# Linear attention whose state is summed in one PSUM bank, its chunks worked through two at a time

## What is computed

```python
# attention: batch 2, heads 8, seq 768, head_dim 64
state = gamma * state + k[t] (outer) v[t]          # one 64x64 state per batch and head
y[t]  = 1/sqrt(64) * q[t] @ state                  # gamma = 1 - 2**(-5-head)
x = y laid out as 1536 tokens x 512
# first feed-forward part, d_ff 2048
h = x @ w_in;  x = (h * sigmoid(1.702 h)) @ w_out
# second, d_ff 1536
xn = x / rms(x) * rms_g
x  = (silu(xn @ w_gate) * (xn @ w_val)) @ w_out
```

## Time and profile before

| | |
|---|---|
| three runs | 586.87, 587.14, 587.15 us; median 587.14 |
| profiled execution | 587.46 us, of which the span of the core's instructions is 585.6 |
| attention, until the first feed-forward matmul | 0 to 55.26 us |
| feed-forward parts | 55.26 to 585.60 us |
| mean granted clock of TensorE | 0.997 |

### The profile page before, as it was taken

How to read it: one execution, slowest core, us unless ns; L and a number is a source line. 1 busy time by engine, 2 the same in 40 slices (tenths; PEclk the granted TensorE clock), 3 DMA queues, 4 the chain that set the end, 5 groups by cost and what they waited for, 6 DMA issues and landing times.

```text
span 585.6 us, 9221 instructions
## 1 busy us (share of the span) xinstructions
PE 575.1 (98%) x3558; PEld 552.0 (94%) x3558; DVE 356.0 (61%) x472; ACT 307.8 (53%) x533; POOL 169.2 (29%) x187
## 2 busy tenths in 40 slices
PE   6999999999999999999999999999999999999997
PEld 6888999999999999999999999998889999998886
DVE  3599555667334666876426768668764666667332
ACT  1556666744325766654337655563544555564321
POOL 2674444000122452000123453410060544420000
PEclk8999999999999999999999999999999999999999
DMA  8990122321211222322202222223213322223202
GB/s 324 347 315 29 58 69 72 109 86 59 73 37 36 73 73 72 109 73 72 67 8 72 73 73 73 72 73 108 73 37 103 114 72 73 73 72 109 72 0 107
DMA packets 24363, 52.83 MB, mean 90 GB/s; under 512 B 1920, under 2 KB 2048, under 8 KB 24320
## 3 DMA queue, kind: packets, MB, share of 16 engines
q1 hardware_dynamic: 23744, 50.93, 26.9%
q10 hardware_dynamic: 576, 1.32, 0.6%
HBM read 49.09 MB, written 3.15 MB: 89 GB/s over the span
## 4 chain that ended last, share of the span: by engine, by line
PE 95%; DVE 2%; DMA 2%; issue 1%; SPq 0%; ACT 0%
PE bank L470 39%; PE bank L420 17%; PE bank L422 17%; PE bank L423 17%; DMA arena<-attn_in 2%; PE bank L394 1%; PE bank L363 1%; PE bank L388 1%; DVE arena L823 1%; PE bank L373 1%; DVE arena L841 1%; PE bank L511 0%; DVE x_lo L723 0%; DVE w_lo L714 0%; DVE t L736 0%
## 5 line engine op out<-in xcount | busy, mean ns | idle before, releaser
L420 PE MATMUL bank<-x_hi,w_hi 128*128 128x384 f32 x560 | 187.3, 334 | 0.0
L423 PE MATMUL bank<-x_hi,w_lo 128*128 128x384 f32 x560 | 187.1, 334 | 0.0
L422 PE MATMUL bank<-x_lo,w_hi 128*128 128x384 f32 x560 | 187.1, 334 | 0.0
L714 DVE TENSOR_TENSOR w_lo<-raw,w_hi 128x512 fp32r<-128x512 f32 (+2 forms) x148 | 145.9, 1001 | 50.9 <-ACT w_hi L543 50.7
L975 POOL TENSOR_TENSOR raw<-raw 128x256 f32<-128x256 f32 x40 | 31.9, 796 | 324.1 <-DMA raw<-w 324.1
L543 ACT ACTIVATE w_hi<-raw 128x512 fp32r<-128x512 f32 (+2 forms) x148 | 109.0, 763 | 18.5 <-PE bank L423 10.2
L420 PEld LDWEIGHTS bank<-x_hi,w_hi 128*128 128x128 f32 x560 | 105.1, 188 | 0.1
L422 PEld LDWEIGHTS bank<-x_lo,w_hi 128*128 128x128 f32 x560 | 105.1, 188 | 0.1
L423 PEld LDWEIGHTS bank<-x_hi,w_lo 128*128 128x128 f32 x560 | 105.1, 188 | 0.0
L573 ACT ACTIVATE g_hi<-arena 128x768 fp32r<-128x768 f32 x56 | 47.5, 848 | 103.1 <-PE bank L470 103.1
L749 DVE TENSOR_TENSOR g_lo<-arena,g_hi 128x768 fp32r<-128x768 f32 x56 | 55.2, 986 | 75.2 <-ACT g_hi L573 75.2
(11 more groups left out here) (70 smaller groups left out, 591.0 us busy)
## 6 DMA issues: line engine op xcount, KB each, us to landing
raw<-w SPq DMA_DIRECT2D x68, 512.0 KB, 3.5
arena<-attn_in SPq DMA_DIRECT2D x22, 512.0 KB, 6.7
out<-x SPq DMA_DIRECT2D x1, 1536.0 KB, 7.8
out<-x SPq DMA_DIRECT2D x6, 256.0 KB, 2.0
arena<-attn_in ACTq DMA_DIRECT2D x2, 512.0 KB, 8.1
arena<-tables SPq DMA_DIRECT2D x1, 512.0 KB, 6.7
arena<-tables ACTq DMA_DIRECT2D x1, 256.0 KB, 10.6
ident<-ident_in SPq DMA_DIRECT2D x1, 64.0 KB, 11.4
```

The costliest lines, as they stand in the source:

```text
L420: pe.matmul(dst, w_hi[q][:, w], x_hi[:, x], start=start and kk == 0, stop=False, skip_group_check=True)
L422: pe.matmul(dst, w_hi[q][:, w], x_lo[:, x], start=False, stop=False, skip_group_check=True)
L423: mm = pe.matmul(dst, w_lo[q][:, w], x_hi[:, x], start=False, stop=kk == 1, skip_group_check=True)
L714: dve.tensor_tensor(w_lo[q % 3][:, dst], src, w_hi[q % 3][:, dst].bitcast(F32), ALU.subtract)\
```

## The change

- The state is no longer carried from chunk to chunk. The products of a batch are summed in one PSUM bank (bank 6 for the first batch and 7 for the second) with the matmuls' own accumulation: k is decayed with a table that grows by gamma to the minus 128 from chunk to chunk (`k_table`), and the sum is scaled back by gamma to the 128 c when it is read out (`g_table`). ScalarE reads it out (`new_state`), in one copy of 256 columns for a batch's first chunk and in four activations of 64 columns for the others, into a state of 256 columns without zero blocks. Cross becomes eight matmuls of 64 rows by 64 columns.
- The further tables are made on the chip: two rows of the table are loaded as broadcasts to 128 partitions at the head of ScalarE's queue, their product is inverted by a power on GpSimd and refined, and ten small VectorE instructions in all make the rest.
- The mask product is one instruction over 1,024 columns.
- All engines go through the chunks by pairs. TensorE: scores(a), scores(a+1), cross(a), cross(a+1), products(a+1), outputs(a), outputs(a+1), products(a+2).
- At the start, SP loads chunk 1 before the mask and the first weights before the constants; the splits, sums and lowerings for the feed-forward part have other places, and T2 comes later in their order.

```diff
-UPPER = {True: (B11, B21, T3, T1, T2, B22, T4), False: (B11, B21, T1, T2, B22, T3, T4)}
+UPPER = {True: (B11, B21, T3, T1, B22, T2, T4), False: (B11, B21, T1, T2, B22, T3, T4)}
...
             load(0)
+            load(1)
             sp.dma_start(table[:, T_MASK:T_Q], tables[:, T_MASK:T_Q]).then_inc(mask_in, 16)
-            load(1)
+            load_kv(2)
             load(2)
-            load_kv(2)
             load(3)
             load_kv(3)
+            load_weights(0)
...
+            for a in range(SLOTS, STEPS, 2):
+                for b in (a, a + 1):
+
+                    sp.wait_ge(scores_done, b - SLOTS + 1)
+                    if (b - SLOTS) % CHUNKS > 0:
+                        sp.wait_ge(q_decayed, cross_at(b - SLOTS) + 1)
+                    load(b)
+                for b in (a, a + 1):
+                    sp.wait_ge(y_done, b - SLOTS + 1)
+                    load_kv(b)
+                if a == 8:
+                    load_weights(1)
...
+            def new_products(a):
+
+                r, m = a % SLOTS, state_at(a)
+                g, c = chunk_of(a)
+                if c == CHUNKS - 1:
+                    return
+                v = slot[r][:, 1536:2048]
                 pe.wait_ge(kv_in[r], 16 * (a // SLOTS) + 16)
+                pe.wait_ge(k_decayed, m + 1)
+                if c > 0:
+                    pe.wait_ge(state_done, m)
+                for p in range(PAIRS):
+                    for h in range(2):
+                        mm = pe.matmul(val[g][64 * h:64 * h + 64, cols(p, 64)],
+                                       k_dec[m % 2][:, cols(2 * p + h, 64)], v[:, cols(2 * p + h, 64)],
+                                       start=c == 0 and p == 0, stop=c == CHUNKS - 2, skip_group_check=True)
+                mm.then_inc(kv_done, 1)
+
+            def from_state(a):
+                par, x = a % 2, cross_at(a)
                 if a >= 2:
                     pe.wait_ge(y_copied, a - 1)
+                if a % CHUNKS > 0:
                     pe.wait_ge(q_decayed, x + 1)
                     pe.wait_ge(state_done, x + 1)
                     for p in range(PAIRS):
+                        for h in range(2):
+                            rows = slice(64 * h, 64 * h + 64)
+                            mm = pe.matmul(gate[par][rows, cols(p, P)], state[x % 2][rows, cols(p, 64)],
+                                           q_dec[x % 2][rows, cols(p, P)], start=p == 0, stop=False,
+                                           skip_group_check=True)
                     mm.then_inc(cross_done, 1)
...
+            for a in range(0, STEPS, 2):
+                scores(a)
+                scores(a + 1)
+                if a == 0:
+                    new_products(0)
+                    from_state(0)
+                    from_chunk(0)
+                    from_state(1)
+                    new_products(1)
+                else:
+                    from_state(a)
+                    from_state(a + 1)
+                    new_products(a + 1)
+                    from_chunk(a)
+                from_chunk(a + 1)
+                if a + 2 < STEPS:
+                    new_products(a + 2)
...
+            for k, row in enumerate((first_row, next_row)):
+
+                at_ = (CHUNK - 2) * k
+                act.dma_start(row, tables[at_:at_ + 1, T_K:T_K + HEADS].to_broadcast([P, HEADS])).then_inc(rows_in, 16)
             act.dma_start(table[:, 0:T_MASK], tables[:, 0:T_MASK]).then_inc(decay_in, 16)
...
+            def new_state(a):
+                g, c = chunk_of(a)
+                if c == CHUNKS - 1:
+                    return
+                m = state_at(a)
+                act.wait_ge(kv_done, m + 1)
+                if m >= 2:
+                    act.wait_ge(cross_done, m - 1)
+                if c == 0:
+                    ins = act.activation(state[m % 2], val[g][:, 0:256], ACT.Copy)
+                else:
                     for p in range(PAIRS):
+                        ins = act.activation(state[m % 2][:, cols(p, 64)], val[g][:, cols(p, 64)], ACT.Copy,
+                                             scale=g_table[c][:, p:p + 1])
+                ins.then_inc(state_done, 1)
+
+            act.wait_ge(decay_set, 2 * CHUNKS - 1)
+            for a in range(0, STEPS, 2):
+                if a == 4:
                     split_x(0, B11)
                     split_x(0, B21)
                     split_w(0, 0)
                 elif a == 6:
+                    split_w(0, 1)
                     split_x(0, T3)
+                elif a == 8:
                     split_x(0, T1)
+                    split_w(0, 2)
+                    split_x(0, B22)
+                elif a == 10:
                     split_x(0, T2)
+                if a == 0:
+                    new_state(0)
+                    copy_y(0)
+                new_state(a + 1)
+                if a > 0:
+                    copy_y(a)
+                copy_y(a + 1)
+                if a + 2 < STEPS:
+                    new_state(a + 2)
...
             def masked(a):
                 dve.wait_ge(scores_done, a + 1)
+                dve.tensor_tensor(prob[a % 2], twin[a % 2][:, :], table[:, T_MASK:T_Q], ALU.mult)\
+                   .then_inc(probs_done, 1)
+
             dve.wait_ge(mask_in, 16)
+            for a in range(0, STEPS, 2):
+                masked(a)
+                masked(a + 1)
                 if a == 4:
                     lower_x(0, B11)
+                elif a == 8:
+                    sum_x(0, T2)
+                if a == 4:
                     lower_x(0, B21)
+                    lower_w(0, 0)
                 elif a == 6:
                     sum_x(0, T1)
                 elif a == 8:
                     lower_x(0, T1)
                     lower_w(0, 1)
+                if a == 8:
+                    lower_x(0, T3)
+                elif a == 10:
                     lower_x(0, T2)
                     lower_x(0, B22)
                     sum_x(0, T4)
                     lower_w(0, 2)
...
+            pool.wait_ge(decay_set, 1)
+            pool.wait_ge(one_set, 1)
+            pool.tensor_tensor(power, growth, minus_one, ALU.pow).then_inc(inverted, 1)
             pool.wait_ge(decay_in, 16)
             decay_k(0)
             pool.wait_ge(q_table_in, 16)
+            pool.wait_ge(decay_set, 2 * CHUNKS - 1)
+            for a in range(0, STEPS, 2):
+                for b in (a, a + 1):
+                    if b % CHUNKS > 0:
+                        decay_q(b)
+                for b in (a + 1, a + 2):
+                    if b < STEPS and b % CHUNKS < CHUNKS - 1:
+                        decay_k(b)
+                if a in (2, 4):
+                    weight_sum(0, a - 2)
+                    weight_sum(0, a - 1)
```

More of the change, by code:

```diff
@@ L100, in transformer_kernel @@
         k_dec = [part(512) for _ in range(2)]
-        state = [part(512) for _ in range(2)]
-        state_dec = [part(512) for _ in range(2)]
+        state = [part(256) for _ in range(2)]
+        k_table = [table[:, T_K:T_K + HEADS]] + [part(HEADS) for _ in range(1, CHUNKS - 1)]
+        g_table = [None, table[:, T_G:T_G + PAIRS]] + [part(PAIRS) for _ in range(2, CHUNKS - 1)]
+        first_row, next_row = part(HEADS), part(HEADS)
+        growth, rest, power = part(HEADS), part(HEADS), part(HEADS)
+        minus_one = part(HEADS)
         used[0] = 0
@@ L107, in transformer_kernel @@
         m5 = [part(HALF) for _ in range(2)]
-        bank = [ctx.enter_context(nc.psum_tensor(f"bank{i}", [P, 512], F32)) for i in range(8)]
+        twin = [ctx.enter_context(nc.psum_tensor(f"twin{i}", [P, 1024], F32)) for i in range(2)]
+        bank = [twin[i // 2][:, 512 * (i % 2):512 * (i % 2) + 512] for i in range(4)]
+        bank += [ctx.enter_context(nc.psum_tensor(f"bank{i}", [P, 512], F32)) for i in range(4, 8)]
         acc, gate, val = bank[0:4], bank[4:6], bank[6:8]
@@ L396, in outputs @@
                                        prob[par][:, 512 * h + P * p:512 * h + P * p + P],
-                                       start=not cross and p == 0, stop=True, skip_group_check=True)
+                                       start=a % CHUNKS == 0 and p == 0, stop=True, skip_group_check=True)
                 mm.then_inc(y_done, 1)
@@ L625, in _, with copy_y @@
             act.wait_ge(decay_in, 16)
-            for a in range(STEPS):
-                par, m = a % 2, state_at(a)
+            def copy_y(a):
                 g, c = chunk_of(a)
@@ L816, in _ @@
             dve.tensor_copy(ones_r[:, :], ones[:, :])
-            for b in range(2):
-                dve.memset(state[b], 0.0).then_inc(zeroed, 1)
+            dve.wait_ge(rows_in, 32)
+            dve.tensor_tensor(growth, first_row, next_row, ALU.mult).then_inc(decay_set, 1)
+            dve.wait_ge(inverted, 1)
+            dve.wait_ge(decay_set, 1)
+            dve.tensor_tensor(rest, growth, power, ALU.mult).then_inc(decay_set, 1)
+            dve.wait_ge(decay_set, 2)
```

(47 more changed lines are left out.)

90 lines of the change are left out of this document (18 added, 72 removed).

## The result

Measured side by side, the changed kernel takes 589.77 us (median of 7 runs, 588.24 to 590.46) and the kernel before 587.15 (7 runs, 586.87 to 589.40). The ratio of the means, 589.56 and 587.70, is 1.0032, with a 95% interval of 1.0016 to 1.0048, so the kernel is slower by a little, clear of noise. The prediction said no change, 587.1; its range, up to 590.0, holds the median.

A forecast was written before the change was run, and what follows sets the result against it. TensorE was taken to bound the kernel, with only attention's 55.26 us affected. 21.8 + 32.1 = 53.9, plus 0.85 clock and 0.4 hand-overs, gave 55.2; with feed-forward at 530.34, no change: 587.1 us, range 583.0 to 590.0.

The forecast's parts named there:

- The beat: Attention after products(2): 35.2 us of old groups, less 4.0 and 0.6, plus a 1.5 wait, 32.1; full pair 6.7.
- Changing form: TensorE's groups: a new tile form costs about 0.2 us; like groups side by side save 4.0 us, bounds 0 and 4.0.
- Cross on 64x64 tiles: Cross groups: eight 64x64 matmuls, two to a pair, save 0.07 us a group, 0.6 over 9 groups.
- the rival in which the halves take turns: Cross: halves writing one PSUM bank don't pair, +0.9 us on 10 groups, +8 in all, 595, slower; chance 0.05.
- The start: ScalarE's queue: q table lands at 17.1 us instead of 12.7, delaying decay_q(1) and cross(1); products(2) end at 21.8.
- The broadcasts: Head of ScalarE's queue: 144 packets each, 2.1 to 2.3 us each, 4.4 for both, delaying everything behind them.
- The chain of eleven small instructions: VectorE at the start: ten small steps, with GpSimd's power, done by about 11.6 us before kv(0), costed at nothing.
- The clock: Cross(1) to products(2) at the start: half speed after idle time costs 0 to 1.7 us.
- the middle: Clock term at the start: 0.85 us taken, between 0 and 1.7.
- the end: Pairs 8 and 10: VectorE's 3.6 us of lowering spill over by 0.5; feed-forward operands in time, 530.34 us kept.
- Pair 6: Chunks 6 and 7: ScalarE's split of T3 ahead of new_state(7) makes TensorE wait 1.5 us at products(8).

The follow-up runs named there:

- b1: Changed kernel with TensorE's order scores(a), cross(a), scores(a+1), cross(a+1) in each pair but the first; ratio 1.0064 to the kernel before.
- b3_before_rows: Kernel before with the two row broadcasts at the head of ScalarE's queue, read only by a wait of VectorE; ratio 1.0071 to the kernel before.
- a2_filler: Changed kernel with 18 unread matmuls on ones before products(0) and 12 before cross(1); ratio 1.0006 to the kernel before.
- a4_vec_order: Changed kernel with VectorE's lowering of T3 moved behind B22's in pair 10, and T4's sum ahead of the lowerings there; ratio 1.0000 to the kernel before.
- d1_short_decay: Changed kernel with GpSimd's decay of q for chunks 10 and 11 cut to 8 of 512 columns; ratio 0.9991 to the kernel before.
- c1: Changed kernel with GpSimd's third and fourth weight sums moved ahead of decay_k(6); ratio 1.0019 to the kernel before.
- a3: Changed kernel with ScalarE's split of T4 behind the first copy of m1, low-half waits counted in VectorE's actual order; ratio 1.0008 to the kernel before.

## Why the prediction was wrong

It said: the gain in the beat is eaten by the start, 55.2 us of attention against 55.26, and 530.34 behind it. Measured are 56.50 and 531.50.

- **The beat: right.** Changing form costs 0.17 to 0.2 us (b1), full pairs take 6.71 and 6.70 us (predicted 6.7), pair 4 takes 6.24, and TensorE's waits for the state update are gone. Cross on 64x64 tiles pairs its halves in one bank: 26.87-24.97 = 1.90 us for two groups. So the rival in which the halves take turns has fallen. The Trainium skill, TensorEngine Tiling (Array Packing), "Gotcha 1: PSUM Pressure", says that different row tiles can't use one bank at the same time; for row halves that also write different partitions these rows don't agree.
- **The start: right in mechanism, its terms off.** The broadcasts were put at 4.4 us; they cost 4.0 in b3_before_rows, and the q table of the changed kernel landed at 16.4 where 17.1 was expected. The turns are one for one, but not at a steady 62 to 70 packets a microsecond: ScalarE's queue moved 30 from 3 to 4 us, 107 from 6 to 7 and 120 from 7 to 8, with 4 KB packets on the other queue all the time. What sets that speed no run here shows. kv(0) landed at 11.9 us (issued at 2.13, 9.8 to landing), 1.0 earlier than reckoned, and decay_k(0), which waits for it and for no further table, began at 12.03; the profile names VectorE's last small instruction (L894) instead, which ended at about the same time. The chain of eleven small instructions (not ten) was done at 11.97 for 11.6. It cost nothing, as reckoned, since cross(1) waited for the q table until 17.80.
- **The clock: the middle was the wrong choice.** The text had both ends, 0 and 1.7 us, and took 0.85. a2_filler shows 1.75 us for the four groups, at the dear end. This is 0.9 us of the miss, of which the early q table gave back 0.6: products(2) end at 22.99 for 22.65.
- **The step that failed is the end.** The prediction wrote that "VectorE's 3.6 us of lowering in pair 8 spill into pair 10 by 0.5 us, before its first mask at 1.1", and that "none of its first operands comes later than its reader". The spill was 3.0 us (52.98 against the pair's start at 49.96). The 3.6 us were the undisturbed price of the sum for T2 and three lowerings; with a decay of k and two of q beside them on GpSimd they took 6.24 (46.74 to 52.98). L737 at 2.03 us and L723 at 1.58, each with GpSimd beside it, stood in the trace of before. The spill gave 0.8 us in the last pair (6.54, where a4_vec_order has 5.77) and 1.16 us in the feed-forward part, which I had as untouched. d1_short_decay shows the cause.
- **Pair 6: the size right, the place wrong.** I had 1.5 us at products(8), for ScalarE's split of T3. The pair took 7.32 us, as reckoned, but 1.03 of the wait stood at cross(7), for GpSimd, and only 0.16 at products(8). That the number fits is partly luck. With GpSimd's wait gone (c1) most of it comes back at products(8), but decay_k(8) ends there within 0.1 us of ScalarE's read, so that ScalarE alone would have held the pair is not shown.

By places, the 2.5 us between the 588.0 measured and the 585.5 reckoned (55.2 + 530.34) are: 0.3 until products(2) have ended, 0.2 in the pairs from 22.99 to 49.96 (26.97 us against 26.4 of groups and wait and the 0.4 for hand-overs), 0.8 in the last pair (6.54 for 5.7 of groups) and 1.2 in the feed-forward part. So four fifths of the miss lie at the end. What stays open is why the loads of k and v land when they do: decay_k(10), which waits for one, began at 47.57 us in the changed kernel's profile and at 48.15, 48.86, 49.35 and 49.82 in those of a4, d1, c1 and a3, and such a landing can cost TensorE 1.5 us.

## What to carry to other kernels

Look for what the new order puts behind one transfer, and at how many turns stand ahead of that transfer in its queue: two broadcasts of 4 KB cost 4.2 us, more than the 2.5 us of waits for VectorE that the change took away, and moving one line in that queue gave 3 us. Cost an instruction of VectorE with two SBUF inputs by what it takes beside GpSimd, not by its best row (2.03 us for 0.95 here), and follow a late engine to the first operands of the next stage. Where a wait has no releaser or an unlikely one, look in the kernel for what that instruction waits for and find which of these ended just before. Groups of matmuls of one tile form belong side by side.

## What the runs showed of the hardware beyond that

- VectorE and GpSimd slow each other only in some instructions: lowerings with both inputs in SBUF go from 0.95 to 2.03 us, while the mask product, with one input in PSUM, takes 2.34 to 2.36 for two whatever GpSimd does. The Trainium skill, GPSIMD Engine Reference, "1. Specifications", has GpSimd's SBUF interfaces as shared with VectorE, with contention for instructions with two SBUF inputs; d1_short_decay and these rows agree.
- A power on GpSimd over 8 columns took 1.66 us, and a VectorE instruction over 8 columns 0.17, with some 0.2 from one to the next that needs it.
- Idle matmuls that hold TensorE's clock up do not by themselves make the runs agree: with them the kernel before still covers 586.29 to 589.64 us over 12 runs, and c1_pool_sums without them covers 589.31 to 590.65.
